# Expert 0's second part counted up to the capacity, its early rows on buffers of their own, router products woven into the up blocks

## The reference, cut to what matters

```python
logits = x @ w_gate
expert_idx = np.argmax(logits, axis=1)
...
gate_w = probs[np.arange(N), expert_idx]
...
for i in range(N):
    e = expert_idx[i]
    if counts[e] < capacity:
        disp[e, counts[e]] = x[i]
        pos[i] = counts[e]
        counts[e] += 1
        keep[i] = True
h = np.maximum(np.einsum('ecd,edf->ecf', disp, w1), 0.0)
y = np.einsum('ecf,efd->ecd', h, w2)
...
    if keep[i]:
        out[i] = gate_w[i] * y[expert_idx[i], pos[i]]
```

## Time and profile before

| | us |
|---|---|
| median of 3 runs | 443.85 (442.56 to 444.22) |
| the profiled execution | 443.4 |
| its span | 441.7 |
| PE busy | 416.1 (94%) |
| PEld busy | 399.1 (90%) |
| DVE busy | 258.0 (58%) |
| POOL busy | 228.5 (52%) |
| ACT busy | 198.1 (45%) |

### The profile page before, as it was taken

The page is one execution under the profiler, slowest core; times in us unless marked ns, Lnnn a source line. Parts: engine busy times, 40 slices in busy tenths (PEclk is TensorE's granted clock), DMA queues, the critical chain, the costliest instruction groups (busy, mean ns, idle before and its releaser), DMA issues.

```text
span 441.7 us, 9365 instructions
## 1 busy us (share of the span) xinstructions
PE 416.1 (94%) x3270; PEld 399.1 (90%) x3270; DVE 258.0 (58%) x533; ACT 198.1 (45%) x454; POOL 228.5 (52%) x239
## 2 busy tenths in 40 slices
PE   6799999999999999999999999999699999999892
PEld 5688889999999999999999998899699999998672
DVE  6888866766435333454347665827085775825950
ACT  2789943341311113111233333436638687536840
POOL 3999716454323533144355671504917495527952
PEclk9999999999999999999999999999979999999998
DMA  7996034536970100000003361186664776807400
GB/s 250 398 358 199 3 114 134 165 91 215 355 282 1 54 1 0 0 18 36 0 1 106 97 207 38 44 274 243 180 198 135 244 217 213 284 26 227 160 29 10
DMA packets 34339, 61.89 MB, mean 140 GB/s; under 512 B 4798, under 2 KB 27310, under 8 KB 34288
## 3 DMA queue, kind: packets, MB, share of 16 engines
q1 hardware_dynamic: 31280, 55.92, 39.0%
q0 software_dynamic: 3008, 5.29, 3.5%
HBM read 47.92 MB, written 15.18 MB: 143 GB/s over the span
## 4 chain that ended last, share of the span: by engine, by line
PE 50%; PEld 19%; issue 8%; DVE 7%; POOL 6%; ACT 5%; DMA 3%; PEldq 0%; POOLq 0%; ACTq 0%; DVEq 0%
PE bank L1353 20%; PE bank L1368 20%; PEld bank L1545 9%; PEld bank L1583 8%; POOL w_low L626 3%; ACT scores L672 3%; DMA out<-y_out,token 2%; PE bank L1483 2%; PE bank L1474 2%; PE bank L1320 1%; DVE scores L950 1%; PEld bank L1607 1%; PEld bank L1512 1%; PE bank L1284 1%; ACT w_high L655 1%
## 5 line engine op out<-in xcount | busy, mean ns | idle before, releaser
L549 POOL TENSOR_TENSOR g_low<-act_full,g_high 128x384 fp32r<-128x384 f32 x63 | 63.7, 1011 | 114.8 <-ACT g_high L701 114.8
L701 ACT ACTIVATE g_high<-act_full 128x384 fp32r<-128x384 f32 x64 | 33.7, 526 | 150.1 <-DVE act_full L1014 137.5
L1353 PE MATMUL bank<-x_split,w_high 128*128 (+1 forms) x384 | 98.4, 337 | 0.0
L1008 DVE TENSOR_SCALAR neg<-bank,alpha_sb 128x384 f32<-128x384 f32 x64 | 39.3, 613 | 70.9 <-PE bank L1353 70.8
L626 POOL TENSOR_TENSOR w_low<-w_raw,w_high 128x384 fp32r<-128x384 f32 x48 | 50.0, 1072 | 43.1 <-ACT w_high L793 43.1
L1353 PEld LDWEIGHTS bank<-x_split,w_high 128*128 128x128 f32 x384 | 69.1, 188 | 0.2 <-issue 0.2
L1368 PE MATMUL bank<-w_high,g_high 128*128 128x384 f32 x189 | 65.3, 345 | 0.6 <-POOL g_low L549 0.6
L1353 PE MATMUL bank<-x_split,w_low 128*128 (+1 forms) x192 | 64.5, 336 | 0.0
L1368 PE MATMUL bank<-w_high,g_low 128*128 128x384 f32 x189 | 63.8, 338 | 0.0
L1368 PE MATMUL bank<-w_low,g_high 128*128 128x384 f32 x189 | 63.8, 338 | 0.0
L927 DVE TENSOR_TENSOR w_low<-w_raw,w_high 128x384 fp32r<-128x384 f32 x44 | 32.1, 732 | 22.9 <-ACT w_high L655 22.8
(11 more groups left out here) (164 smaller groups left out, 858.7 us busy)
## 6 DMA issues: line engine op xcount, KB each, us to landing
w_raw<-chunks SPq DMA_DIRECT2D x96, 192.0 KB, 3.7
w_raw<-chunks SPq DMA_DIRECT2D x32, 384.0 KB, 3.4
rk_in<-att_rk SPq DMA_DIRECT2D x12, 704.0 KB, 6.3
routed_rows<-fill SPq DMA_DIRECT2D x1, 5211.0 KB, 17.7
xe<-routed_rows SPq DMA_DIRECT2D x7, 579.0 KB, 4.3
v_in<-att_v SPq DMA_DIRECT2D x12, 200.0 KB, 6.0
out<-fill SPq DMA_DIRECT2D x1, 2304.0 KB, 23.9
x_split<-x_split POOLq DMA_DIRECT2D x18, 48.0 KB, 2.6
```

What stands on the lines that cost most here:

```text
L549: pool.tensor_tensor(gl[:, f % 4, :], act_full[:, f % 2, :], gh[:, f % 4, :].bitcast(f32), ALU.subtract).then_inc(s_gl, 1)
L701: act.activation(gh[:, f % 4, :], act_full[:, f % 2, :], ACT.Copy).then_inc(s_gh, 1)
L1008: dve.tensor_scalar(neg[:, f % 2, :], h, 0.0, alpha_sb[:, f:f + 1], ALU.min, ALU.mult)\
L1353: last = mm(bank[f % 4][:, 0:G], a[:, f, w], x[:, kc, bass.ds(g * G, G)], start=kc == 0 and i == 0, stop=kc == KC - 1 and i == 2)
```

## The change

It does seven things.

1. `counts[0]` becomes min(CNT[0], CAP) + base_0, one instruction in place of one.
2. `early_token` and `early_gate`, two small tiles, take the place of `token[:, 1]` and `gate[:, 1]` in the early part. The DVE wait for `s_outa` in `keep_meta(1)` goes. ACT's wait for it before expert 1's first `y_copy` (L815) stays, as `y_out[:, 1]` is still shared.
3. POOL issues the two `early_scatter` after `split_low` of chunk 28 and before those of chunks 29 to 31. They stood behind these three and eight `split_low1`.
4. In the branch of 128 rows or fewer, ACT and DVE split chunks 29 to 31 at the end of expert 0's work and no longer near its beginning. The other branch keeps them in place.
5. On PE the router of the last group is laid differently into the early ups: two thirds of `early_up(0)`, two tiles of `turn_rows`, the last third, the third tile, two thirds of `early_up(1)`, `logits`, the last third, `turn_logits`, `early_up(2)`, `positions`, `early_up(3)`.
6. On DVE `choose` comes before `early_low(1)`.
7. On ACT `gate_exp` comes after two `early_relu` and not three.

```diff
+    early_token = mlp.take("early_token", [P, ET], i32)
+    early_gate = mlp.take("early_gate", [P, ET], f32)
...
+            for c in range(2 * NF - 4 - DEFER, 2 * NF - 3):
+                split_low(c)
+            for i in reversed(range(ET)):
+                early_scatter(i)
+            for c in range(2 * NF - 3, 2 * NF):
+                split_low(c)
...
-                if e == 0:
-                    for i in reversed(range(ET)):
-                        early_scatter(i)
...
-            for f in range(3):
+            for f in range(2):
                 early_relu(f)
             gate_exp(NG - 1)
-            early_relu(3)
+            for f in range(2, 4):
+                early_relu(f)
...
                 with act.If(rows[e] < P + 1):
                     if e == 0:
                         xe_high(0, 2, bank[6])
-                        for c in range(2 * NF - 3, 2 * NF):
-                            split_high(c)
...
                     act.sem_inc(s_fc[1], 2)
+                    if e == 0:
+                        for c in range(2 * NF - 3, 2 * NF):
+                            split_high(c)
...
             early_low(0)
             logits_copy(NG - 1)
+            choose(NG - 1)
             early_low(1)
-            choose(NG - 1)
...
-                if e == 1:
-                    dve.wait_ge(s_outa, 16 * ET)
...
-            dve.tensor_tensor(counts[0:1, 0:1], CNT[:, 0:1], base_0[0:1, :], ALU.add).then_inc(s_cnti, 1)
+            dve.scalar_tensor_tensor(counts[0:1, 0:1], CNT[:, 0:1], float(CAP), base_0[0:1, :], ALU.min, ALU.add)\
+               .then_inc(s_cnti, 1)
...
                     low2(3, 4, 5, 6, 7)
+                    if e == 0:
+                        for c in range(2 * NF - 3, 2 * NF):
+                            split_low(c)
...
-            early_up(0)
-            turn_rows(q)
-            early_up(1)
+            early_up(0, (0, 1))
+            turn_rows(q, (0, 1))
+            early_up(0, (2,))
+            turn_rows(q, (2,))
+            early_up(1, (0, 1))
             logits(q)
+            early_up(1, (2,))
+            turn_logits(q)
             early_up(2)
-            turn_logits(q)
+            positions(q)
             early_up(3)
-            positions(q)
             early_up(4)
```

More of the change, by code:

```diff
@@ L610, in y_scatter @@
                     oob_is_err=False).then_inc(done, 16)
-            for c in range(2 * NF - 4 - DEFER, 2 * NF):
-                split_low(c)
             def early_scatter(i):
@@ L617, in early_scatter @@
                 pool.indirect_dma_start(
-                    out=out, out_offset=bass.IndirectOffsetOnAxis(ap=token[:, 1, i:i + 1], axis=0),
+                    out=out, out_offset=bass.IndirectOffsetOnAxis(ap=early_token[:, i:i + 1], axis=0),
                     in_=y_out[:, 1, i, :], in_offset=None, bounds_check=N - 1,
                     oob_is_err=False).then_inc(s_outa, 16)
+            for c in range(2 * NF - 4 - DEFER, 2 * NF - 3):
[4 more added lines that the diff above has]
+                split_low(c)
             def split_low1(e, f):
@@ L763, in early_y @@
                 act.activation(y_out[:, 1, i, :], bank[4 + i][:, 0:DM], ACT.Copy,
-                               scale=gate[:, 1, i:i + 1]).then_inc(s_ayo, 1)
-            for f in range(3):
+                               scale=early_gate[:, i:i + 1]).then_inc(s_ayo, 1)
+            for f in range(2):
                 early_relu(f)
             gate_exp(NG - 1)
-            early_relu(3)
+            for f in range(2, 4):
+                early_relu(f)
             for f in range(4, 4 + DEFER):
@@ L1167, in _ @@
             dve.wait_ge(s_xea, 16)
-            dve.tensor_copy(token[:, 1, 0:ET], xe[:, 1, 0:ET, DM:DM + 1].rearrange("p a b -> p (a b)"))
-            dve.tensor_copy(gate[:, 1, 0:ET], xe[:, 1, 0:ET, DM + 1:ROW].rearrange("p a b -> p (a b)"))\
+            dve.tensor_copy(early_token[:, :], xe[:, 1, 0:ET, DM:DM + 1].rearrange("p a b -> p (a b)"))
+            dve.tensor_copy(early_gate[:, :], xe[:, 1, 0:ET, DM + 1:ROW].rearrange("p a b -> p (a b)"))\
                .then_inc(s_metaa, 1)
@@ L1370, in products, with turn_rows @@
                 return last
-            def turn_rows(q):
-                for i in range(GT):
+            def turn_rows(q, tiles=range(GT)):
+                for i in tiles:
                     pe.wait_ge(s_x2, q * GT + i + 1)
@@ L1461, in _, with early_up @@
                 last.then_inc(s_tile if i < GT - 1 else s_step, 1)
-            def early_up(f):
+            def early_up(f, kcs=range(KC)):
                 pe.wait_ge(s_wl1, NF + f + 1)
@@ L1470, in early_up @@
                     pe.wait_ge(s_agl, f - 3)
-                for kc in range(KC):
+                for kc in kcs:
                     w = slice(kc * P, (kc + 1) * P)
@@ L1475, in early_up @@
                                   start=kc == 0 and i == 0, stop=kc == KC - 1 and i == 2)
-                last.then_inc(s_ah, 1)
+                if kcs[-1] == KC - 1:
+                    last.then_inc(s_ah, 1)
             def early_down(i, f):
```

## The result

The changed kernel takes 435.62 us (median of 4 runs, 435.41 to 436.16), the kernel before 443.72 in the same session; the ratio is 0.9823, 95% interval 0.9801 to 0.9844. The forecast was 429.4 with a range of 427.0 to 433.0. It is faster, as was said, but by 8 us (1.8%) and not by 14.

The account below looks back on a forecast made before the run. TensorE, busy 94% of the span, was taken as the bound, so only fewer columns or fewer standstills help. Router 0.4, expert 0 7.3 and expert 1 6.3 make 14.0 us off 443.4: 429.4 us, range 427.0 to 433.0.

Parts of the forecast that it names:

- the term for expert 0: Expert 0 on PE: one tile in place of two takes 11.0 us instead of 18.33, a gain of 7.3 us.
- over 12 us: Sign of being wrong: expert 0 takes over 12 us in the new profile.
- the 19.2 of the sum: Expert 1 on PE: without the early-scatter wait it takes 19.2 us instead of 25.46, a gain of 6.3 us.
- the term of 1.3 us for lateness: Expert 1: 0.7 us idle from ACT's late relu plus some 0.6 from DVE's low parts slowed beside POOL.
- the row I took (1.12): DVE in expert 1: a `split_low2` takes 1.12 us beside POOL, against 0.55 alone.
- The 2.0 us that the prediction gives for this rule: Expert 1: if DVE's low parts wait out whole POOL splits, three banks cost some 2.0 us; sum 430.1.
- The router: PE from first early up to first early down, 11.83 us before: the new order gains 0.4 us (0 to 0.9).
- At nothing: Parts counted as worth no time: the count instruction, the early scatter's place, two copies to new buffers, `gate_exp`.
- Downstream: From expert 2 on nothing changes its neighbour; all shifts together, the waits near 411 and 419 us too.
- A new deep stall in expert 1: Rival: ACT or POOL comes 5 us late, PE falls to 1.2 GHz, expert 1 keeps 25.46; 435.7 us, chance 0.10.

Follow-up runs that it names:

- run 1: The changed kernel with expert 0's branches taken out of TensorE's program: one-tile code stands straight, its two- and three-tile code left out; 442.12 us.
- run 2: The changed kernel with TensorE's two-tile code placed before the one-tile code for all experts; 434.23 us.
- run 6: The changed kernel with 32 never-executed transposes added at the end of expert 0's two-tile code on TensorE; 436.26 us.
- run 10: The changed kernel with two-tile code first on TensorE for experts 0 to 4, DVE's order left as it was; 431.36 us.
- run 11: The changed kernel with DVE's wait for the early rows in the output put back before expert 1's token copy; 435.37 us.
- run 7: The changed kernel with SyncE waiting for expert 0's first down step before it loads expert 2's w2; 435.88 us.
- run 12: The changed kernel with the router of the last group laid as before on PE, DVE and ACT; 436.47 us.
- run 8: The changed kernel with two-tile code first for experts 0 and 1, and in expert 1 DVE's low parts of expert 2's w2 four steps later; 434.78 us.
- run 9: The changed kernel with two-tile code first for experts 0 to 4, and in expert 1 DVE's low parts of expert 2's w2 four steps later; 429.78 us.
- run 5: The changed kernel with two-tile code first in TensorE's program for experts 0 and 1 alone, total code length unchanged; 433.31 us.

## Why the prediction was wrong

**The step that failed** is the term for expert 0: "I take 11.0 us, with ends of 10.6 and 11.8". It measured 16.12, 5.1 of the 6.2 us by which the sum missed; the prediction itself had named "over 12 us" here as a sign of being wrong. The work was right, to a few hundredths: 11.03 in run 1 and 11.00 in run 2. What was left out is the supply of code. Two waits for TensorE's instructions, 1.90 and 2.79 us with their ends, and after them 1.2 GHz at expert 1's beginning. The sum counted instructions by their durations and no instruction by its address, though after expert 0's one-tile code TensorE jumps over the two-tile code, 108 products by the program, where before it jumped over the 38 of the one-tile code. The 74 products of the third tile, behind both, are skipped before and after.

**It could have been seen.** I read expert 5's last 1.00 us as a wait for POOL, as the profile says. The DMA view of the kernel before, the 1.2 us from 408.6, has this row:

```profile
q8 instruction: 1, 0.02, 5.8%
```

There is none in the 1.1 us before it. It began at 408.64 and PE went on at 411.53, 2.89 us later, like the gaps after the change. POOL's last split for expert 6 had ended at 403.1. Expert 5 takes the same path that expert 0 was now to take, one-tile code and then the two jumps, and in the sum I took those 1.00 us off as another's affair. The Trainium skill has the rule too: "Runtime: NRT & Kernel Launch", section "Instruction fetch mechanics", says that instructions come in blocks of 16 KiB, fetched ahead in sequence alone, and that a taken branch out of the blocks at hand stalls until its block is fetched. The traces agree, in the size of the packets (0.51 MB in 31) and in run 6, where dead code moved the gaps; I had weighed only the port that DVE and POOL share.

**Expert 1.** The stall for the early scatter went, as forecast, and 25.46 fell to 19.92. But this is not the 19.2 of the sum: it holds some 2 us of the low clock, and as the gap gave ACT, DVE and POOL time to catch up, hardly any of their lateness. Where the gap is away, expert 1 takes 20.6 (runs 1, 2, 10). So the term of 1.3 us for lateness was half of the 2.7 that those runs show, and that 19.92 came so near to 19.2 is luck. `relu(1, 0)` at 14.8 us and the 1.0 to 1.4 us of DVE beside POOL were right; what I missed is who waits at the end of the ups. `expert_down(1, 1)` waits in `turned` for two tiles of `xe_low(2, ...)`, which stand behind DVE's slow low parts: 1.32 us more.

**POOL and DVE.** The Trainium skill's rule ("SBUF — State Buffer", section "Who interferes with whom") made a split of 1.0 us and the low part's own 0.55 add up, 1.55 at most. The first three of run 2 have 1.44, 1.02 and 1.05: one is nearer to the rule, two are a little under the row I took (1.12). The 2.0 us that the prediction gives for this rule was low by its own numbers: three banks at 0.41 + 1.55 = 1.96 us in place of 1.08 are 2.6, before ACT's 0.7.

**The router** gave 11.5 against 11.83 us from the first early up to the first early down, 0.3 for 0.4. "At nothing" held for the early scatter, which POOL issued at 293.76, and for the wait that goes with the buffers (run 11); the instruction of the count and `gate_exp` no run tests by themselves. "Downstream" held for experts 2 to 7: 105.1 us for 105.0.

**The rivals.** "A new deep stall in expert 1" gave 435.7 us and 0.10, and the time came out there, but its cause (ACT or POOL 5 us late) is not what happened. No rival asked whether TensorE's own program arrives.

## What to carry to other kernels

In this kernel a branch chosen at run time cost by where its code lay. Before changing which way it goes, find the transfers of the instruction queue in the DMA view and match them with PE's gaps called "issue", or put down to an engine that had long been done. Put the code that will run where a straight path or a short jump reaches it, and expect that any edit in front shifts the gaps of all code behind: judge it by several placements, and not by one build. And a wait that is taken away also gave the other engines time to catch up: look at who is late next, up to the last wait of the stage.

## What the runs showed of the hardware

- From the start of a needed 16 KB transfer of instructions to PE's next product it was 2.6 to 3.3 us in ten gaps of six kernels (2.80 and 2.90 after the change, 2.89 before it, 2.64, 3.05 and 2.69 in run 1, 2.75 in run 2, 3.28 in run 6, 2.72 and 2.83 in run 7); the first gap of run 12 has 2.48. How soon the transfer begins depends on the load of the DMA engines: 1.3 us after the first product behind the jump with the weights' loads held back, 2.5 with a DMA share of 1.07.
- 32 products that never run moved two gaps of 1.9 and 2.8 us into one of 6.0. Taking expert 0's unused branches out of TensorE's program made the kernel 6.5 us slower.
- Kernels with such gaps can spread widely: 431.4 to 436.3 us in run 8 and 436.7 to 444.3 in run 1, against 429.0 to 431.8 in run 9, whose path has few. But the changed kernel, with two of them, spread by 0.8 us in four runs. That the gaps themselves differ from one execution to the next is not shown, as each kernel has one trace.
- PE's clock fell to 1.2 GHz in the second of two gaps of 1.9 and 2.8 us with 1.1 us of work between, and stayed full through the single gap of 1.54 us in run 5. The length of the gap alone does not tell: after 1.97 us in run 8 and 2.67 in run 2 it fell, after 2.94 in run 1 (at 399.06) it stayed at 1.00.
